# Startup order, table copy in DRAM and row products of a kernel that transforms and applies two layers, on Trainium2

## The reference, cut to what matters

```python
X = np.fft.fft(x, axis=1)            # x: 4 batches, 3008 rows, 256 columns
x = np.fft.fft(X, axis=2).real
h = x @ w_in;  g = relu(h) ** 2;  y = g @ w_out          # 256 -> 2048 -> 256
h = y @ w2_in; g = h * np.cos(h); out = g @ w2_out       # 256 -> 2048 -> 256
```

## Time and profile before

| | us |
|---|---|
| median of 3 runs | 2002.7 (2002.55 to 2003.88) |
| the profiled execution | 2002.4 |
| its span | 2000.6 |
| DVE busy | 1432.8 |
| ACT busy | 1261.3 |

### The profile page before, as it was taken

The page is one execution under the profiler, slowest core; times in us unless marked ns, Lnnn a source line. Parts: engine busy times, 40 slices in busy tenths (PEclk is TensorE's granted clock), DMA queues, the critical chain, the costliest instruction groups (busy, mean ns, idle before and its releaser), DMA issues.

```text
span 2000.6 us, 21409 instructions
## 1 busy us (share of the span) xinstructions
PE 1938.1 (97%) x8500; PEld 1599.5 (80%) x8500; DVE 1432.8 (72%) x1663; ACT 1261.3 (63%) x1318; POOL 0.2 (0%) x4
## 2 busy tenths in 40 slices
PE   6599999999999999999999999999999999999998
PEld 5487888788788888878888878888888888888887
DVE  6576876776787687676687678767667667677665
ACT  4475765665676576576576566557667567567554
POOL 0000000000000000000000000000000000000000
PEclk9699999999999999999999999999999999999999
DMA  8730112111311311200011121020000000000000
GB/s 308 264 94 12 53 50 81 59 59 42 117 34 38 109 50 40 88 29 6 22 52 50 66 83 60 29 89 6 1 31 6 0 26 7 6 11 11 1 11 21
DMA packets 36228, 106.08 MB, mean 53 GB/s; under 512 B 3544, under 2 KB 14040, under 8 KB 35680
## 3 DMA queue, kind: packets, MB, share of 16 engines
q1 hardware_dynamic: 35904, 95.43, 13.9%
q10 hardware_dynamic: 224, 9.29, 1.4%
HBM read 86.17 MB, written 27.82 MB: 57 GB/s over the span
## 4 chain that ended last, share of the span: by engine, by line
PE 89%; DVE 5%; ACT 3%; DMA 2%; issue 1%; SPq 0%; ACTq 0%; DVEq 0%
PE ps L865 88%; DVE gh L796 1%; DMA ab<-scratch_a 1%; ACT u L640 1%; ACT u L635 1%; DVE kbuf L826 1%; DVE u L832 1%; ACT osb L586 1%; DVE u L836 1%; DVE u L849 1%; DMA scratch_a<-est 0%; DVE u L831 0%; ACT kbuf L645 0%; DMA wst<-w1i 0%; ACT gh L639 0%
## 5 line engine op out<-in xcount | busy, mean ns | idle before, releaser
L865 PE MATMUL ps<-gh,wo 128*128 128x502 f32 x4608 | 1128.7, 393 | 17.4 <-DVE gh L796 10.5
L865 PEld LDWEIGHTS ps<-gh,wo 128*128 128x128 f32 x4608 | 870.8, 189 | 213.8 <-DVE gh L796 15.4
L865 PE MATMUL ps<-y,wi 128*128 128x502 f32 x2304 | 556.9, 391 | 3.0 <-DVE u L849 1.9
L865 PEld LDWEIGHTS ps<-y,wi 128*128 128x128 f32 x2304 | 435.0, 189 | 91.9 <-DVE u L849 2.3
L836 DVE TENSOR_TENSOR u<-kbuf,ps 128x1004 f32<-128x1004 int32 x192 | 230.6, 1201 | 356.7 <-ACT kbuf L645 356.7
L796 DVE TENSOR_TENSOR gh<-u,gh 128x1004 fp32r<-128x1004 f32 x384 | 460.1, 1198 | 3.3 <-ACT u L640 2.0
L645 ACT ACTIVATE kbuf<-ps 128x1004 int32<-128x1004 f32 x192 | 193.9, 1010 | 360.1 <-PE ps L865 359.1
L635 ACT ACTIVATE u<-u 128x1004 f32<-128x1004 f32 x192 | 200.8, 1046 | 208.3 <-DVE u L832 207.8
L865 PE MATMUL ps<-eo,weo 128*128 128x502 f32 x1152 | 296.1, 392 | 23.7 <-DVE u L832 19.2
L865 PEld LDWEIGHTS ps<-eo,weo 128*128 128x128 f32 x1152 | 218.5, 190 | 70.3 <-DVE u L832 19.9
L826 DVE SCALAR_TENSOR_TENSOR kbuf<-ab,w,ps 128x502 f32<-128x502 f32 x192 | 141.6, 737 | 151.5 <-PE ps L865 131.2
(11 more groups left out here) (69 smaller groups left out, 334.1 us busy)
## 6 DMA issues: line engine op xcount, KB each, us to landing
ring<-scratch_t SPq DMA_DIRECT2D x72, 378.0 KB, 3.5
xin<-x SPq DMA_DIRECT2D x36, 512.0 KB, 3.3
out<-osb SPq DMA_DIRECT2D x24, 502.0 KB, 3.6
scratch_t<-tables ACTq DMA_DIRECT2D x2, 4536.0 KB, 19.5
raw<-scratch_eo SPq DMA_DIRECT2D x11, 502.0 KB, 4.8
scratch_eo<-est SPq DMA_DIRECT2D x14, 376.5 KB
stage_t<-tables SPq DMA_DIRECT2D x6, 756.0 KB, 17.4
tab_odd<-scratch_t SPq DMA_DIRECT2D x2, 2268.0 KB, 27.3
```

The costliest lines, as they stand in the source:

```text
L865: op = pe.matmul(out_, a, b, start=start and i == 0, stop=stop and i == len(todo) - 1)
```

## The change

The start gets another order on every engine: `x128` and the first rows of batch 0 are loaded ahead of the constants, the others among the pieces of W1, whose fourth piece comes last. DVE sums rows ahead of the low parts of W1. The fourth product of W1 runs behind the three row products, in other banks of PSUM. The odd table's copy is issued ahead of the first row copy on ACT, and the even one's at the end of up item 15 of tile 0; both are written as 768 rows of 1512 words instead of one block. Row product 3 runs behind item 8, 4 behind item 11, and 5 behind the flush. The pieces of W2-out are split in pairs in mixes 0 to 3. The later row products run three pieces behind each of mixes 2, 3, 5 and 6, and their rows are taken in mixes 4 and 7. The diff, but for unchanged lines:

```diff
@@ -93,7 +93,7 @@
-ROW_ITEMS = {7: 3, 10: 4, 13: 5}
+ROW_ITEMS = {8: 3, 11: 4}
 
@@ -104,7 +104,7 @@
-    items.append("flush")
+    items += ["flush", Item("row", r=5)]
     items += [Item("mix", 0, 0, i) for i in range(NM)]
@@ -188,12 +188,13 @@
-                for i, at_ in enumerate((A_WO1 + 12288, A_WI2 - 4096))]
+                for i, at_ in enumerate((A_WO1 + 8192, A_WO1 + 12288))]
     cin, = area(A_Y1 + 7040, A_GH, ("cin", [P, 2, 4 * P + 2], F32))
...
-    wps, w128ps, early = [ps[2], ps[3], ps[0], ps[2]], ps[1], [ps[3], ps[0], ps[1]]
+
+    wps, w128ps, early = [ps[2], ps[3], ps[0], ps[0]], ps[1][:, 1, BANK - 2 * NF:], [ps[3], ps[1], ps[2]]
     yb, hb = ps[0:2], ps[2:4]
@@ -265,21 +266,19 @@
-        if it.kind == "mix" and it.sign == 0 and it.t in MADE_IN and it.index >= 2:
+        if it.kind == "mix" and it.sign == 0 and it.t in MADE_IN and it.index in (2, 3, 5, 6):
             b, phase = MADE_IN[it.t]
...
-            first = 2 * (it.index - (5 if odd else 2))
-            return number[b, phase, int(odd)], range(first, first + 2)
+            first = 3 * (it.index - (5 if odd else 2))
+            return number[b, phase, int(odd)], range(first, first + 3)
         return None
...
-        if it.kind == "mix" and it.sign == 0 and it.t in MADE_IN and it.index == 5:
-            return number[(*MADE_IN[it.t], 0)]
-        if it.kind == "up" and it.t - 1 in MADE_IN and it.index == 0:
-            return number[(*MADE_IN[it.t - 1], 1)]
+        if it.kind == "mix" and it.sign == 0 and it.t in MADE_IN and it.index in (4, 7):
+            return number[(*MADE_IN[it.t], int(it.index == 7))]
         return None
@@ -296,12 +295,15 @@
-        n = it.index + 2 + (NF if it.kind == "mix" else 0)
-        return n if it.t == 0 and it.sign == 0 and n < NW else None
+        if it.kind == "up" and it.t == 0 and it.index + 2 < O2:
+            return [it.index + 2]
+        if it.kind == "mix" and it.t == 0 and it.sign == 0:
+            return range(O2 + 2 * it.index, min(O2 + 2 * it.index + 2, NW))
+        return []
 
...
-        return it.index - 1 if it.kind == "up" and it.t == 0 and 1 <= it.index <= 2 else None
+        return it.index if it.kind == "up" and it.t == 0 and it.index < 2 else None
 
@@ -394,14 +396,19 @@
+        sp.dma_start(lx[:, :, :, :], x128).then_inc(lx_in, 16)
+        load_x0(0)
         sp.dma_start(cin[:, :], consts).then_inc(c_in, 16)
-        sp.dma_start(lx[:, :, :, :], x128).then_inc(lx_in, 16)
-        for q in range(WQ):
-            load_w1(q)
-        for kt in range(KT):
-            load_x0(kt)
-        for n in range(2 * KT):
+        load_w1(0)
+        load_x0(1)
+        load_w1(1)
+        load_w1(2)
+        load_x0(2)
+        for n in range(KT):
             load_even_table(n)
+        for n in range(KT, 2 * KT):
+            load_even_table(n)
+        load_w1(3)
         for n in range(4):
@@ -416,10 +423,10 @@
-        for n in range(6, 13):
+        for n in range(6, 14):
             load_split(n)
...
-        for n in range(13, O2):
+        for n in range(14, O2):
             load_split(n)
@@ -439,8 +446,6 @@
-            if t - 1 in MADE_IN:
-                store_rows(number[(*MADE_IN[t - 1], 1)])
             store(t - 1, 0)
@@ -462,6 +467,7 @@
+                store_rows(number[(*MADE_IN[t], 1)])
         store(NT - 1, 0)
@@ -505,10 +511,14 @@
+        def copy_tables(odd):
+            act.dma_start(scratch_t[odd].rearrange("p t o h k -> (p t) (o h k)"),
+                          tables[odd].rearrange("p t o h k -> (p t) (o h k)")).then_inc(tab_st[odd], 16)
+
         def split_high(n):
...
-            if n == 6:
+            if n == 4:
                 act.wait_ge(odd_lo, 2)
@@ -516,40 +526,39 @@
-        w1_high(0)
-        w1_high(1)
         act.wait_ge(lfolded, 2)
...
+        w1_high(0)
         even_high(0)
+        w1_high(1)
+        even_high(1)
         w1_high(2)
...
-        w1_high(3)
         weo_high(1)
...
-        even_high(1)
+        even_high(2)
+        w1_high(3)
         table_parts(1)
...
-        weo_high(3)
-        act.activation(w128[:, :], w128ps[:, 0, 0:2 * NF].rearrange("p (i o) -> p i o", o=2)[:, :, 0],
-                       ACT.Copy).then_inc(w128_out, 1)
-        for n in range(3, 2 * KT):
+        for n in range(KT, 2 * KT):
             table_parts(n)
-        even_high(2)
+
+        copy_tables(1)
         copy_odd_rows(0)
-
-        act.dma_start(scratch_t[1], tables[1]).then_inc(tab_st[1], 16)
         copy_odd_rows(1)
...
+        split_high(0)
         act.wait_ge(rows_out, 3)
...
-        split_high(0)
         split_high(1)
-        act.dma_start(scratch_t[0], tables[0]).then_inc(tab_st[0], 16)
+        weo_high(3)
+        act.activation(w128[:, :], w128ps.rearrange("p (i o) -> p i o", o=2)[:, :, 0],
+                       ACT.Copy).then_inc(w128_out, 1)
 
@@ -593,12 +602,14 @@
-            if splits_in(it) is not None:
-                if splits_in(it) == O2:
+            for n in splits_in(it):
+                if n == O2:
                     act.wait_ge(rows_done, INSIDE)
-                split_high(splits_in(it))
+                split_high(n)
             if odd_step(it) is not None:
...
+            if it.t == 0 and it.kind == "up" and it.index == NF - 1:
+                copy_tables(0)
 
@@ -609,7 +620,7 @@
-                    act.wait_ge(rows_done, INSIDE)
+                    act.wait_ge(rows_done, number[0, 1, 1] + 1)
                     y1_high(0, 0)
@@ -738,34 +749,33 @@
+        fold_first(0)
         w1_low(0)
+        even_low(0)
+        fold_first(1)
         w1_low(1)
-        fold_first(0)
+        even_low(1)
         w1_low(2)
-        even_low(0)
+        fold_first(2)
         dve.wait_ge(wsp_lo, 3)
-        fold_first(1)
+        weo_low(0)
+        even_low(2)
+        weo_low(1)
         w1_low(3)
-        even_low(1)
+        take_rows(0)
         dve.wait_ge(wsp_lo, WQ)
-        weo_low(0)
-        weo_low(1)
-        fold_first(2)
         weo_low(2)
-        even_low(2)
-        take_rows(0)
-        weo_low(3)
         take_rows(1)
-        dve.wait_ge(w128_out, 1)
         for phase in range(2):
...
+        split_low(0)
         take_rows(2)
...
-        split_low(0)
         split_low(1)
+        weo_low(3)
 
@@ -851,8 +861,8 @@
-            if splits_in(it) is not None:
-                split_low(splits_in(it))
+            for n in splits_in(it):
+                split_low(n)
             if odd_step(it) is not None:
@@ -871,7 +881,8 @@
-                pe.wait_ge(weo_lo, 1)
+                pe.wait_ge(weo_lo, 3)
+                pe.wait_ge(rows_out, 2)
             for e in range(2):
@@ -879,7 +890,7 @@
-                        op = pe.matmul(w128ps[:, 0, at_:at_ + 2], wsp[half][:, q % 2, kt, i * P:(i + 1) * P],
+                        op = pe.matmul(w128ps[:, at_:at_ + 2], wsp[half][:, q % 2, kt, i * P:(i + 1) * P],
                                        cs[:, 0, 4 * P:], start=kt == 0 and half == 0, stop=kt == 1 and half == 1)
@@ -907,21 +918,20 @@
-        for q in range(WQ):
+        for q in range(3):
             w1_product(q)
...
-        pe.wait_ge(weo_lo, 3)
         for kt in range(KT):
...
-        pe.wait_ge(w128_out, 1)
         for kt in range(KT):
...
+        w1_product(3)
 
@@ -949,10 +959,7 @@
-                pe.wait_ge(w128_out, 1)
-                pe.wait_ge(weo_lo, WQ)
-            elif it.c == 1:
-                pe.wait_ge(rows_out, 1)
+                pe.wait_ge(rows_out, EARLY)
             if it.kind == "up":
@@ -977,7 +984,8 @@
-                    pe.wait_ge(rows_out, EARLY)
+                    pe.wait_ge(w128_out, 1)
+                    pe.wait_ge(weo_lo, WQ)
                 if it.t == 0 and it.index % 2 == 0:
```

## The result

The changed kernel takes 1973.7 us (median of 4 runs, 1972.2 to 1974.6) against 2002.8; the ratio is 0.9853 with a 95% interval of 0.9836 to 0.987. The profiled execution's span is 1972.0 instead of 2000.6.

A forecast was written before the change was run, and what follows sets the result against it. TensorE was busy 97% of the span, so only its idle time could be won, chiefly 29 us on two small transfers at the start. Terms -14.2 (start), -1.1 (row product 5), -5.8 (threes) gave -21.1: 1981.6 us, range 1974 to 1991.

The forecast's parts named there:

- The laying out of the start: Start: new engine orders laid end to end with old durations; first `kbuf` at 51.8, 19.1 us earlier.
- the threes: Later tiles: row products in groups of three instead of two remove TensorE idle time in six tiles, -5.8 us.
- where it issues the odd copy: ACT's chain at the start: odd copy issued at 39.6, after six table parts, against 37.9 before.
- piece 6: W1-out's seventh piece, tile 0: lands at 75.6 behind the odd table, wanted at 70.3; ACT waits 5.3 us.
- the clock: Ahead of item 4: TensorE standing still some 4 us lowers the granted clock, +1.6 us.
- small packets: Table copies on ACT's queue: rows of 6,048 B expected to go out as 3 KB packets; `ab` ready at 50.2.
- rival C: Start: turns stay long, `ab` lands at 60, first `kbuf` gains only 11 us; 1984.8 us, chance 0.15.
- The price of a turn: DMA queues alternate row by row, each turn costing the other queue's packet: 2.36 us large, 0.15 to 0.3 small.
- Rival B: Start: nothing late in DMA, piece 6 lands by 70.3; -26.0 us, 1976.7 us, chance 0.15.
- Row product 5: Moved behind the flush, it covers TensorE's 1.10 us wait ahead of the first mix: -1.1 us, bounds 0 and -3.
- the pairs: Last weight pieces split in pairs, mixes 0 to 3: cost 0, up to 0.5 us for each of four mixes.

The follow-up runs named there:

- e2: Changed kernel with a wait for all six table parts ahead of the odd copy, issuing it at 39.81: 1980.1 us, 0.9891 of before.
- e9: Changed kernel with the odd copy written ahead of five table parts and a `weo` piece: 1973.2 us in one run.
- e4: Changed kernel with the odd copy held back by a wait for all six table parts and `scratch_t` rows padded by 128 B: 1980.2 us in one run.
- e10: Changed kernel with the even table's copy back at the start, behind `w128`'s copy on ACT: 1984.5 us in one run.
- e1: Changed kernel with the table copies written as one block again: 1973.3 us in one run.
- e5: Kernel before with only the row products in threes, their rows taken in mixes 4 and 7: 1995.1 us, 0.9954 of before.
- e8: Kernel before with only `scratch_t` padded, so both table copies go in rows of 6,048 B: 2000.8 us in one run, beside 2003.1.
- e7: Kernel before with only the even table's copy moved behind up item 15 of tile 0: 1986.7 us in one run, beside 2003.1.
- e6: Changed kernel with the row products in twos again and their rows taken where they were: 1981.0 us in one run.
- e14: Kernel before with only the odd copy moved up, behind the high part of W1's fourth piece: 2000.1 us in one run, beside 2001.6.
- e3: Changed kernel with `scratch_t` rows padded by 128 B so the copy's rows cannot be joined: 1972.0 us in one run.
- e13: Changed kernel with row product 5 back among the up items, behind item 14: 1974.5 us, 0.9867 of before.
- e12: Changed kernel with three ACT and DVE steps moved into idle time and `scratch_t` rows padded by 128 B: 1972.0 us, 0.985 of before.
- e11: Changed kernel with W1's fourth piece later on ACT, and a `weo` piece and odd sums earlier on DVE: 1973.2 us, 0.9857 of before.

## Why the prediction was off

**Right at its end, in part by errors that cancel.** The laying out of the start gave the first `kbuf` at 51.8; measured 51.58. Its late links fit (the first row product's rows 41.4, measured 41.06; product 3 at 43.5 to 48.2, measured 43.35 to 48.1). Its early ones do not: the first product began at 14.47 instead of 15.6 and the row products at 31.40 instead of 32.4 (32.2 by the sum's own terms), and then ACT waited 1.58 us for W1's fourth piece and TensorE 0.59 for a table part, which the laying out had not. The idle time that the threes remove, 5.8 us, was right: TensorE's idle time in a plain one of the six tiles went from 1.8 to 0.67, and the `eo` split's 0.8 stayed (160.56 busy in 162.03).

**The step that failed: "where it issues the odd copy", 39.6.** The copy stands behind six table parts in ACT's program, and I put it behind them in time. ACT's queue had passed them at 30.8, since none of their waits was open any more. With 39.6 the sum had piece 6 landing at 75.6, 5.3 us late, which made 3.3 us of it, and 1.6 for the clock. In the changed kernel piece 6, issued at 54.23, landed at 66.9, some 3 us ahead of the 70.0 at which ACT wanted it, and both terms, 4.9 us, were nothing. e2 and e9 show both sides: held back, 6.4 us are lost; written earlier, nothing moves.

The trace of before had already shown it. The first row copy (L501) stands ahead of the odd copy (L542) in ACT's program, and yet:

```profile
37.89 0.61 ACTq L542 DMA_DIRECT2D scratch_t<-tables  x1
...
40.30 0.46 ACT L501 ACTIVATE est<-ps 4x377 f32<-4x377 f32 x1
```

The copy is issued 2.4 us before the instruction ahead of it begins, and 0.04 us after the first row product, which that instruction waits for, has ended (37.85).

**Had 39.6 been right, the number would have been near by luck.** e4 has the copy at 39.86 and small packets, and its 1980.2 us are near the forecast of 1981.6. Piece 6 landed at 75.9, as laid out. But `ab`, which the sum had at 50.2, landed at 57.9, so that ACT wanted the piece only at about 76.4 and waited for nothing: the time was lost on `ab`, as in rival C, and not on piece 6. The price for the clock was real where TensorE did stand still: in e10 twelve matmuls took 4.68 us behind 6.74 us of idle, with a granted clock of 0.59 over 86.69 to 91.20, and 2.88 at 1.00 from 92.57 on. The prediction's 1.2 GHz for a clock of 0.50 can be had from the traces as an estimate only: in the kernel before, matmuls of 502 columns started every 432 ns at 0.50 (twelve from 77.33 to 82.52) and every 227 ns at 1.00 (twelve from 84.08 to 86.80); taken as the same 502 columns at half the rate, the 206 ns more make 2.4 columns a ns at 1.00 and 1.2 at 0.50. That a cycle takes one column is assumed in this.

**A premise that was wrong and cost nothing: small packets.** Packets did not change (e1), which I had as rival C with 0.15, and its end, 17.9 us of gain, assumed the copy to run till 57. The price of a turn as the other queue's packet did not hold for small packets either (`ab` took 9.9 us in e4 instead of 5.5). The match of 8 turns by 2.36 us with 19.25 is one number and proves no turns, and that each engine has 8 of the 128 rows was my estimate; the trace of before allows another reading, since the even copy, issued at 48.33, landed 22.0 us later, at 70.3, and `ab` 0.6 us behind it (in e5 0.2). In e8 `ab` landed at 61.3 with the even copy running to 79.4, so with small packets at least `ab` did not wait for the end. No run separates the two readings for large ones. e8's 20 packets against 220 speak against a strict alternation by row, and they and the 165 against 166 behind them prove no grouping either: how an engine shares between two queues was not shown. What ended `ab`'s trouble was the even copy far away (e7: 14.1 us at item 4) and the odd one well under way (store 6.3 us with the copy issued 10.2 us earlier, 8.9 in e2 with 2.3 us).

**Rival B's number without its reason.** B had 1976.7 for "nothing late in DMA" and took piece 6 to be in time; that is what happened, through an early copy. The rest of the way to 1973.7 is in three terms. The threes gave 7.4 instead of 5.8: the idle time as predicted, and TensorE's busy time in such a tile fell from 160.6 to 160.32 us. The page has it in the row matmuls alone:

```profile
L865 PE MATMUL ps<-ring,fa 128*128 128x378 f32 x216 | 43.4, 336 | 0.0
...
L875 PE MATMUL ps<-ring,fa 128*128 128x378 f32 x216 | 41.5, 336 | 0.0
```

The kernels with six groups of them in a tile (before, e6, e7, e14) have 43.4, those with four (the changed one, e3, e5, e13) 41.4 or 41.5. Row product 5 gave 1.3 to 1.5 instead of 1.1. And the clock that fell in the third mix of before's profiled execution and not in the changed kernel's gave 1.4 to 1.5, which is luck and not of the change; the pairs, put at 0 with up to 0.5 for each of four mixes, took about 0.5 back.

**Sum in hindsight, for the two profiled executions.** 18.9 at item 4 (14.1 in e7 with the even copy late alone, and 4.8 more with the new order and the early odd one) + 1.3 + 1.5 - 0.5 + 7.4 = 28.6; 28.6 in the spans. The 18.9 is good to about 1 us only: from the first `kbuf` to item 4's down product it took 25.9 us in the changed kernel's trace and 24.5 in e3's, which has the same order, with granted clocks of 0.79 and 0.96 from 60 to 70.

## What to carry to other kernels

In these runs, the place of a DMA in ACT's program said only which waits it stood behind. It was issued 0.01 to 0.04 us after the last of them had ended (37.89 after 37.85 before, 30.83 after 30.79 in the changed kernel, 39.81 after 39.78 in e2, 30.50 after 30.49 in e9), up to 8.7 us ahead of work that stood before it. Look for that wait in the trace, and use it: here a bulk copy did well where its last wait ended just as the loads before it had landed (30.77; held back to 39.81 it cost 6.4 us), and one that nobody needed soon did well far behind (e7: 1986.7 against 2003.1). Where a small transfer waited beside a large one here, taking the large one away won time (e7: `ab` in 4.8 us instead of 19.25), and cutting it into smaller packets won none (15.7 us for store and load in e4 and in e2; e8: 2000.8 against 2003.1 in single runs). Then ask which transfer is late next. And before a microsecond is put down to an edit, look whether the granted clock differs between the two profiles (0.50 in e6 and 1.00 in the changed kernel from 142 to 144, 4.56 against 3.03 us for the same twelve matmuls).

## What the runs showed of the hardware that was not expected

The two copies inside DRAM, each written as 768 rows side by side, went out as 224 packets, as two blocks did (before, e1); with 128 B between the rows it was 1568, and the odd one took 17.8 us in e3 instead of 17.4, so rows of 6 KB cost little with not much beside them; with `ab` and the weight pieces beside it, it took 19.7 in e4 and e8 instead of 16.8 (e2) and 17.0 (before). Beside such a copy, the store of row product 0 (11.8 KB), read as the time from its issue to that of `ab`, took 5.8 to 6.4 us with small packets (e3, e4, e8, e12). With large ones it took 5.7 to 7.5 where the copy had been issued 8 to 10 us earlier (the changed kernel, e1, e6, e9, e10, e11, e13) and 8.9 to 9.8 where it had been issued 2 to 4 us earlier (before, e2, e5, e7). In e14, with no copy beside it, it took 1.6. ACT issued a DMA up to 8.7 us ahead of the work before it in its program (30.83, with the last table part ending at 39.53). And the granted clock fell in seven of sixteen traces, and did not in the others, behind the same 1.9 us of idle, in e6 and the changed kernel in programs that are the same up to there. Such a fall is worth 0.9 to 1.5 us between two profiles.
